# Soft-capped attention and a squared-ReLU layer: all score tiles of a head pair in one PE visit, slots cut at whole tiles of the hidden layer

## The reference, cut to what matters

```python
# 4 batches, 12 heads, 448 tokens, head size 64
scores = 1/sqrt(64) * q @ k.T
scores = cap * tanh(scores / cap)
attn = softmax(scores)
x = (attn @ v), heads side by side       # 1792 tokens x 768
h = x @ w_in                             # 768 -> 2048
r = maximum(h, 0)
y = (s * r * r + b) @ w_out              # 2048 -> 768
```

## Time and profile before

| what | value |
| --- | --- |
| three runs | 625.71, 625.73, 626.56 us, median 625.73 |
| the profiled execution | 625.9 us |
| its span | 624.0 us |
| PE busy | 617.2 us (99%) |
| DVE busy | 330.9 us (53%) |
| ACT busy | 258.4 us (41%) |
| POOL busy | 46.3 us (7%) |
| chain that ended last | PE 95%, DVE 2%, DMA 1%, issue 1% |

### The profile page before, as it was taken

The page is one execution under the profiler, slowest core; times in us unless marked ns, Lnnn a source line. Parts: engine busy times, 40 slices in busy tenths (PEclk is TensorE's granted clock), DMA queues, the critical chain, the costliest instruction groups (busy, mean ns, idle before and its releaser), DMA issues.

```text
span 624.0 us, 8174 instructions
## 1 busy us (share of the span) xinstructions
PE 617.2 (99%) x3206; PEld 480.3 (77%) x3206; DVE 330.9 (53%) x565; ACT 258.4 (41%) x272; POOL 46.3 (7%) x46
## 2 busy tenths in 40 slices
PE   7999999999999999999999999999999999999998
PEld 3335666777777777777779999999888888888997
DVE  4986999998677677677663332222411121111311
ACT  7885455656555555555413322222411121111220
POOL 0115724700000000000000000000000000000000
PEclk9999999999999999999999999999999999999999
DMA  8432245343222222231014112222522234111501
GB/s 289 143 117 61 87 155 157 108 130 94 72 92 87 76 88 91 71 92 58 29 60 148 59 51 58 70 78 75 175 79 59 66 112 125 48 42 33 165 2 64
DMA packets 31863, 57.17 MB, mean 92 GB/s; under 512 B 3536, under 2 KB 18000, under 8 KB 31824
## 3 DMA queue, kind: packets, MB, share of 16 engines
q1 hardware_dynamic: 31824, 56.64, 28.6%
HBM read 40.11 MB, written 16.52 MB: 91 GB/s over the span
## 4 chain that ended last, share of the span: by engine, by line
PE 95%; DVE 2%; DMA 1%; issue 1%; ACT 0%; SPq 0%; ACTq 0%; DVEq 0%
PE banks L480 13%; PE banks L482 13%; PE banks L481 13%; PE banks L497 12%; PE banks L496 12%; PE banks L498 12%; PE banks L438 8%; PE banks L393 5%; PE banks L352 3%; PE banks L450 2%; PE banks L418 1%; DMA work<-w_in 1%; PE banks L461 1%; DVE e_sum L725 0%; DVE w_lo L707 0%
## 5 line engine op out<-in xcount | busy, mean ns | idle before, releaser
L480 PE MATMUL banks<-x_hi,w_hi 128*128 128x448 f32 x384 | 142.9, 372 | 0.0
L482 PE MATMUL banks<-x_hi,w_lo 128*128 128x448 f32 x384 | 140.7, 366 | 0.0
L481 PE MATMUL banks<-x_lo,w_hi 128*128 128x448 f32 x384 | 140.6, 366 | 0.0
L497 PE MATMUL banks<-x_lo,w_hi 128*128 128x512 f32 (+2 forms) x384 | 139.4, 363 | 0.0
L498 PE MATMUL banks<-x_hi,w_lo 128*128 128x512 f32 (+2 forms) x384 | 139.4, 363 | 0.0
L496 PE MATMUL banks<-x_hi,w_hi 128*128 128x512 f32 (+2 forms) x384 | 139.4, 363 | 0.0
L813 DVE SCALAR_TENSOR_TENSOR x_lo<-e,beside,x_hi 128x512 fp32r<-128x512 f32 (+1 forms) x48 | 32.5, 683 | 115.5 <-ACT x_hi L641 115.5
L480 PEld LDWEIGHTS banks<-x_hi,w_hi 128*128 128x128 f32 x384 | 72.1, 188 | 15.0 <-issue 8.3
L641 ACT ACTIVATE x_hi<-e,beside 128x512 fp32r<-128x512 f32 (+1 forms) x48 | 31.7, 669 | 116.7 <-PE banks L498 116.7
L496 PEld LDWEIGHTS banks<-x_hi,w_hi 128*128 128x128 f32 x384 | 72.1, 188 | 9.0
L497 PEld LDWEIGHTS banks<-x_lo,w_hi 128*128 128x128 f32 x384 | 72.1, 188 | 8.9
(11 more groups left out here) (67 smaller groups left out, 550.0 us busy)
## 6 DMA issues: line engine op xcount, KB each, us to landing
hidden_scratch<-hidden_sb SPq DMA_DIRECT2D x48, 224.0 KB, 1.9
beside<-q_k SPq DMA_DIRECT2D x23, 448.0 KB, 4.0
e<-hidden_scratch SPq DMA_DIRECT2D x32, 256.0 KB, 2.7
e<-w_out SPq DMA_DIRECT2D x16, 384.0 KB, 3.1
work<-w_in SPq DMA_DIRECT2D x22, 256.0 KB, 5.5
v_sb<-v SPq DMA_DIRECT2D x24, 192.0 KB, 2.5
y_t<-beside SPq DMA_DIRECT2D x10, 256.0 KB, 2.1
e<-hidden_scratch SPq DMA_DIRECT2D x16, 160.0 KB, 2.2
```

Source lines behind the costliest of these rows:

```text
L480: nc.tensor.matmul(out, w_hi[:, j, w], x_hi[:, batch % 2, c, :], start=c == 0, stop=False)
L481: nc.tensor.matmul(out, w_hi[:, j, w], x_lo[:, batch % 2, c, :], start=False, stop=False)
L482: last = nc.tensor.matmul(out, w_lo[:, j, w], x_hi[:, batch % 2, c, :], start=False, stop=c == CT - 1)
L497: nc.tensor.matmul(out, w_hi[:, j, w], ring(x_lo, n), start=False, stop=False)
```

## The change

It redraws the slots. Slots end at whole hidden tiles: 2, 2, 3, 2, 2, 3 tiles in slots 6 to 11 and 3, 2, 3, 3, 2, 3 in the slots of the other batches. On PE the last scores follow the first ones directly and go to the two banks of `hid`. The tail scores go to banks 2 and 3, behind the product with v, and get a tanh of their own. PE gets new waits: for `relu_done` before the last scores, for `last_read` before a slot's first hidden tile, for `tails_read` before the first scores of an odd pair. On ACT the two tanhs come before the exponentials, and `split_high` moves from the head of the slot behind them. On DVE `split_low` moves from the head of the slot behind the additions; the slot's first tile is squared before `invert`, all others after it.

```diff
-EARLY = 2 * CT
+EARLY = 2
+FIRST_ENDS = (4, 6, 9, 11, 13, 16)
+ENDS = (3, 5, 8, 11, 13, 16)
...
+        def tiles_beside(batch, c):
+            ends = FIRST_ENDS if batch == 0 else ENDS
+            first = EARLY if batch == 0 else 0
+            return range(ends[c - 1] if c else first, ends[c])
+        def first_tiles(batch):
+            return [tiles_beside(batch, c).start for c in range(PAIRS) if (batch + 1) * PAIRS + c + 1 < ALL] if batch < B - 1 else []
...
+            def free_scores(p):
+                pe.wait_ge(first_read, first_group(p - 1))
+                if p == PAIRS + 1:
+                    pe.wait_ge(last_read, last_group(PAIRS))
+                elif p % 2:
+                    pe.wait_ge(tails_read, tails_group(p - 1))
+            def free_hidden(p):
+                batch, c = divmod(p - 1, PAIRS)
+                pe.wait_ge(relu_done, (batch - 1) * JT + tiles_beside(batch - 1, c).start)
...
             def first_split_scores(p):
                 pe.wait_ge(qk_hi_done, p - SPLIT + 1)
                 pe.wait_ge(qk_lo_done, p - SPLIT + 1)
-                pe.wait_ge(last_read, last_group(p - 1))
+                free_scores(p)
...
+                if c == 0 and j in first_tiles(batch):
+                    pe.wait_ge(last_read, last_group((batch + 1) * PAIRS + first_tiles(batch).index(j) + 1))
...
                 if p + 1 < SPLIT:
                     first_scores(p + 1)
+                    free_hidden(p + 1)
+                    last_scores(p + 1, G1)
                 elif p + 1 < ALL:
                     first_split_scores(p + 1)
+                    free_hidden(p + 1)
+                    last_split_scores(p + 1, G1)
                 values(p)
                 if p % 2:
                     tail_values(p - 1, 2)
-                if p + 1 < ALL:
-                    pe.wait_ge(first_read, first_group(p + 1))
-                    if p % 2:
-                        tail_scores((p + 1) // 2, 0)
-                    bank = 2 if p % 2 else 0
-                    if p + 1 < SPLIT:
-                        last_scores(p + 1, bank)
-                    else:
-                        last_split_scores(p + 1, bank)
-                for chunk in range(*chunks_of(batch - 1, c)):
-                    hidden_chunk(batch - 1, chunk)
+                    if p + 1 < ALL:
+                        pe.wait_ge(first_read, first_group(p + 1))
+                        tail_scores((p + 1) // 2, 2)
+                for j in tiles_beside(batch - 1, c):
+                    for c_in in range(CT):
+                        hidden_chunk(batch - 1, CT * j + c_in)
...
+            def tails_tanh(p):
+                act.wait_ge(tails_done, p // 2 + 1)
+                act.wait_ge(pv_done, products(p - 1))
+                act.wait_ge(e_sum_done, 3 * p)
+                nc.scalar.activation(e[:, G1:G1 + 2, :], scores[:, 2:G1, 0:S], ACT.Tanh, scale=tanh_scale
+                                     ).then_inc(tails_read, 1)
...
-                if SPLIT <= p + 2 < ALL:
-                    split_high(p + 2)
-                if p + 1 < ALL:
-                    first_tanh(p + 1)
-                    exponential(p + 1, 0)
-                if p + 1 < ALL:
-                    last_tanh(p + 1)
-                    exponential(p + 1, 1)
+                if p + 1 < ALL:
+                    first_tanh(p + 1)
+                    last_tanh(p + 1)
+                    exponential(p + 1, 0)
+                    if p % 2:
+                        tails_tanh(p + 1)
+                    exponential(p + 1, 1)
+                if SPLIT <= p + 2 < ALL:
+                    split_high(p + 2)
...
-                if SPLIT <= p + 2 < ALL:
-                    split_low(p + 2)
                 if p % 2:
                     scale_pair(p - 1)
                     scale_pair(p)
                 if p + 1 < ALL:
                     add_first_e(p + 1)
                     add_last_e(p + 1)
-                start, end = chunks_of(batch - 1, c)
-                for j in tiles_in(start, start + 8):
-                    square((batch - 1) * JT + j)
+                if SPLIT <= p + 2 < ALL:
+                    split_low(p + 2)
+                tiles = tiles_beside(batch - 1, c)
+                square((batch - 1) * JT + tiles[0])
                 if p + 1 < ALL:
                     invert(p + 1)
-                for j in tiles_in(start + 8, end):
+                for j in tiles[1:]:
                     square((batch - 1) * JT + j)
```

More of the change, by code:

```diff
@@ L35 @@
 PIECES = CT * FF // PIECE
-CHUNKS = JT * CT
-SHARE = CHUNKS // PAIRS
-EARLY = 2 * CT
+EARLY = 2
+FIRST_ENDS = (4, 6, 9, 11, 13, 16)
+ENDS = (3, 5, 8, 11, 13, 16)
+assert len(ENDS) == len(FIRST_ENDS) == PAIRS and ENDS[-1] == FIRST_ENDS[-1] == JT
 CONSTS = 8
@@ L141, in attention_ffn @@
         last_read = sem("last_read")
+        tails_read = sem("tails_read")
         exp_done = sem("exp_done")
@@ L195, in last_group, with tails_group @@
             return p + 2
[L197 to L206, removed]
+        def tails_group(p):
+            return (p - PAIRS) // 2
+        def tiles_beside(batch, c):
[4 more added lines that the diff above has]
+            return [tiles_beside(batch, c).start for c in range(PAIRS) if (batch + 1) * PAIRS + c + 1 < ALL] if batch < B - 1 else []
         def hidden_tile(n):
@@ L315, in _ @@
                 if p == PAIRS:
-                    for j in tiles_in(0, EARLY):
+                    for j in range(EARLY):
                         store_hidden(j)
-                for j in tiles_in(*chunks_of(batch - 1, c)):
+                for j in tiles_beside(batch - 1, c):
                     store_hidden((batch - 1) * JT + j)
@@ L361, in first_scores @@
                 pe.wait_ge(qk_in[p % QK_SLOTS], qk_loads(p))
-                if p > 0:
+                if 0 < p <= PAIRS:
                     pe.wait_ge(first_read, first_group(p - 1))
@@ L597, in last_tanh @@
                 act.wait_ge(last_done, p + 1)
+                if p > PAIRS:
+                    tile = tile_of(p, FULL - 1, 0)
+                    nc.scalar.activation(e[:, tile:tile + 2, :], hid[:, :, 0:S], ACT.Tanh, scale=tanh_scale
+                                         ).then_inc(last_read, 1)
+                    return
                 if p % 2 == 0:
@@ L612, in last_tanh @@
                 else:
-                    source = banks[:, 0:2, 0:S] if p % 2 else banks[:, 0:4, 0:S]
+                    source = scores[:, :, 0:S]
                 nc.scalar.activation(e[:, group_of(p, 1), :], source, ACT.Tanh, scale=tanh_scale).then_inc(last_read, 1)
+            def tails_tanh(p):
[4 more added lines that the diff above has]
+                                     ).then_inc(tails_read, 1)
             def split_high(p):
@@ L626, in exponential @@
                 act.wait_ge(last_read if group else first_read, last_group(p) if group else first_group(p))
+                if group and p > PAIRS and p % 2 == 0:
+                    act.wait_ge(tails_read, tails_group(p))
                 nc.scalar.activation(e[:, group_of(p, group), :], e[:, group_of(p, group), :], ACT.Exp, scale=cap_c
```

## The result

The median of eight runs was 628.18 us (627.60 to 628.93), against 626.38 (625.71 to 626.77) for the kernel before: ratio 1.0031, 95% interval 1.0022 to 1.0039, so 1.8 to 1.9 us slower. That lies in the stated range (622.5 to 628.8), but 1.5 us above where the forecast put it (626.7). The forecast's own range (625.7 to 628.5) holds the time too, but its mechanism isn't the one that gave it: the granted clock fell, as in the rival that stood at 628.7. The profiled execution took 628.66 us, its span is 626.9 against 624.0.

A forecast was written before the change was run, and what follows sets the result against it. PE's own work was taken as the bound: joins -3.1, slot 10 wait +4.0 and small waits +0.1 sum to +1.0 us, giving 626.7 us on the median of 625.73; stated range 622.5 to 628.8, the forecast's own 625.7 to 628.5.

The forecast's parts named there:

- the rival that stood at 628.7: PE's clock falls to 1.2 GHz in the 4 us wait, costing up to 2.0 us more: 628.7; chance 0.13.
- The wait: PE waits at slot 10 for split_low(11), now behind DVE's scaling and additions: 4.0 us, bounds 3.0 to 4.6.
- a reordering leaves the end of a set in place: In DVE's unbroken queue, 73.6 to 121.2 us, a given set of instructions is done at the old trace's time.
- the swap changes nothing in the sum: On DVE, a square joins the stretch crowded by POOL where split_low left it; the sum stays the same.
- The joins: On PE, one visit to the score products saved in each of slots 6 to 22, 0.20 or 0.18 us each: 3.1 us.
- The last tanh: On ACT, done 0.14 us before PE's hidden tiles in even slots: taken as 0, at most 0.2 in each of nine.
- The odd slots with two tiles: In slots 13 and 19, PE waits 0 to 0.2 us each for split_low on DVE; taken as 0.05.
- the new place of `split_high`: On ACT, it can no longer hold up a tanh while waiting for q and k: worth nothing.

The follow-up runs named there:

- Experiments two: The changed kernel with three hidden tiles in slot 9 and two in slot 11, orders untouched: 622.30 us, ratio 0.9938 to the kernel before.
- five: The kernel before with split_high and split_low moved behind, as in the change, and nothing else: 628.83 us, ratio 1.0045.
- six: The changed kernel with split_low(11) ahead of the additions in slot 9: 623.93 us; then split_low(12) ahead in slot 10 too: 622.08 us.
- experiment three: The changed kernel with 20 extra matmuls, results unused, on PE ahead of the wait at slot 10: 626.06 us, ratio 0.9998 to the kernel before.
- experiments one: The changed kernel with split_high and split_low back at the head of the slot: 624.16 us, ratio 0.9967 to the kernel before.
- seven: The kernel before with the new slot sizes (whole tiles) alone, all orders and banks as before: 630.35 us, ratio 1.0069.

## Why the prediction was right or wrong

**Right in kind.** The reading that PE is the bound and that time can only be lost by making it wait; the place of the loss, slot 10; its releaser, `qk_lo(11)`, read off the old trace as the end of a fixed set of instructions. Experiments two, five and six show it: moving PE's arrival by 3.8 us left the start of slot 10 where it was, and moving this one instruction took the wait away.

**The wait: 4.0 predicted, 4.7 measured**, 0.1 over the upper bound. The same set ended at 122.25, not 121.31: 0.94 later. PE was 0.37 later too (117.68 for 117.31: slots 6 and 7), and 0.1 lies between the end and the start. The 0.94 is DVE's own busy time: 71 instructions take 45.48 us from 73.60 to 121.31 before, and 46.42 from 73.60 to 122.25 after. It is the sum of its meetings with POOL that grew. From 75 us to the end of the set, DVE's instructions take 8.1 us more before, and 8.9 after, than the shortest of their kind in the same trace, of which 7.9 and 8.7 us fall on instructions that overlap one of POOL's. The last `split_low` is one of them (2.14 us for 1.08, beside POOL's piece from 119.32 to 121.31), but the old trace has such a meeting at the end of the set as well. No run changed POOL's work to test this. I said a reordering leaves the end of a set in place. Here that held to 0.94 us. The page "SBUF — State Buffer" of the Trainium skill (Who interferes with whom) has the lock between the two engines, and this trace agrees (2.14 us beside POOL, 1.08 without); my sentence that the swap changes nothing in the sum didn't hold.

**The clock: the step that failed.** I gave it 0.13 and left it out of the forecast, at 2.0 us. It came in all eight runs (mean clock 0.994 to 0.997) and cost 2.65 in the profile, 2.1 in the medians of experiment three. The page "TensorE: Matmul & The Clock Gate" of the Trainium skill (Part 1) says that an idle TensorE falls to half rate, and the runs agree with it: 0.50 in the profile from 122.3 to 126.0, and a full clock where fillers took the place of the standstill. I had written down a wait longer than any before and a rule that speaks of such waits, and should have put most of the chance there. That the rival's 628.7 lies within 0.5 us of the measured 628.18 is partly luck: the wait (by 0.7) and the clock (by 0.65) cost more than it had, and the joins (by 0.3) and the pace (by 1.6) gave back more. It put the loss at 3.0 us over a median of 625.73; the eight runs of the kernel before had 626.38, so that the loss is 1.8.

**The joins: 3.1 predicted, 3.4 measured**, 0.20 a slot for 0.18.

**The pace: not in the prediction.** The change gained 1.6 us in a way that no step had. It hid the size of the rest: without it the result would have been some 3.4 us slower.

**Small terms.** The last tanh had 0.25 us to spare in slot 16 (0.14 predicted). The odd slots with two tiles wait 0.05 us each as predicted. Slot 7 costs 0.2 us that I hadn't: its last scores wait until tile 3 is rectified (done at 75.52, they start at 75.56), and ACT was itself idle for 4.1 us until a store had freed a buffer. And the new place of `split_high`, put at nothing, is worth some 1.6 to 2.3 us: the waits of experiments one and seven show what the old place costs once the slots have new sizes. No run moved `split_high` alone.

## What to carry to other kernels

Where a queue runs without a gap, an instruction moved behind others is done about when the last of them was done in the old trace (0.94 us later here): check this against its user, and check every later user too, since the first wait covers the next. A wait of TensorE, where it bounds the kernel, costs itself and perhaps its clock: put the chance and the price of that into the forecast. Sizes and orders have to be tried together: in the changed kernel one number (a third tile in slot 9) gave as much as a new order for two instructions, but in the kernel before whole tiles alone cost 4.3 us.

## What the runs showed of the hardware

A standstill of PE and its clock, by kernel (the standstill read from one profile of each, the mean clock from every run): 4.6 us, clock below full in 8 of 8 runs (0.994 to 0.997); 3.6 us, 5 of 6; 2.3 us in the kernel before with whole tiles, 3 of 6 (0.997; 631.3 to 631.8 us against 628.9 to 629.4); 2.3 and 2.2 us in two others, 2 of 7 and 1 of 5; 1.6 us and less, none of the 26 runs of four other kernels below 0.999. These are odds for this kernel, where PE works densely before and after the standstill, from few runs each. The clock need not fall within the standstill: in the kernel before with whole tiles PE restarted at 138.95 us, and the granted clock was 1.00 to 139.5, 0.90 from there to 140.0 and 0.50 to 141.0.

Two small DVE copies of one kind (`recips`, L765, kernel before) show what a meeting with POOL can cost: the one that starts at 95.22 us takes 0.16 us, the next, which starts at 95.41 inside a POOL product (95.25 to 96.54), takes 1.16.

Layer 1's matmuls, 448 columns each, follow one another at 202.6 or 206.5 ns, with the granted clock at 1.00, and the pace holds for a whole slot. It was the same in two profiles of one program and different after small changes elsewhere, as far as one profile of each tells: putting `split_low` of one pair ahead in slot 9 turned slots 7 and 8 slow and slot 11 fast. Whole tiles, the place of the splits and the score visit were each tried, and none of them alone decides it.
